# Folding two weight matrices with split fp32r matmuls instead of fp32 ones, beside a routing chain, in a fused attention and mixture-of-experts kernel

## The chip, the cores and the metric

The kernel runs on one NeuronCore of a Trainium2 chip. The metric is the device time of one execution in microseconds, as the median of several runs. The engines are called PE (TensorE, the matrix engine; PEld is its weight load), ACT (ScalarE), DVE (VectorE), POOL (GpSimd) and SP (SyncE, which here only issues DMAs).

## What is computed

Three layers in a row, all float32:

```
S = 768, B = 4, H = 8, D = 48            # linear attention with decay
for t in range(S):
    y[t]  = r[t] @ (state + (u*k[t]) outer v[t])
    state = w * state + k[t] outer v[t]
x = y as [3072, 384]                     # tokens by features
skip   = x @ w_skip <= 0                 # such tokens pass unchanged
e      = argmax(x @ w_gate)              # one of 8 experts
x     += softmax(x @ w_gate)[e] * (relu(x @ w1[e]) @ w2[e])
out    = (((x @ wm1) * (x @ wm2)) @ w3) @ w_out     # w3 1024x1024, w_out 1024x384
```

The kernel never multiplies a token by w3: it first computes the product w3 @ w_out ("the fold"), 1024x384, and multiplies by that.

## The kernel before

The program has three stages on the time axis: attention (0 to about 121 us), routing (about 122 to 155 us: which token goes to which slot of which expert), experts (to about 291 us), and the gated layers (to the end). All five instruction queues run through them without a barrier between the first three.

**The fold** (class `Fold`, lines 40 to 102) is spread over the end of attention, the routing, and the seams of the experts, to give PE work while it would wait for others. It goes by chunks of 128 rows of w3, i = 0 to 7. For each: `load` (SP, line 59) brings the chunk into one of three buffers `w3_in`; `turn` (PE, line 69) transposes it in eight pieces into two PSUM banks; `turned` (ACT, line 77) copies these to `w3T` as float32 in two halves of 512 columns; `product` (PE, line 84) multiplies the eight pieces of `w3T` by the eight row blocks of w_out (`wo`) and sums in one bank, 128x384; it can be called by quarters of two pieces; `taken` (ACT, line 99) copies the result to `wf`. `product` uses plain fp32 matmuls, which the trace shows as two records each, so 16 for a product. Chunk 0 is turned and multiplied in attention, chunks 1 to 4 and half of 5 in the routing, the rest later.

**The rest of the kernel** uses "split" operands where it multiplies: ACT writes the fp32r rounding of a value (`hi`), DVE subtracts it from the value and writes the remainder (`lo`), and PE does three fp32r matmuls, hi by hi, hi by lo, lo by hi. So do the experts (line 1277 first layer, line 1293 second layer, the latter with 128x128 stationary and 384 moving columns) and the gated layers (lines 1523 and 1538).

**The order of work around the change** is written out by hand, one queue per engine:

- SP: behind attention's last stores of x it waits for the last logits (`s_lg`, line 286), loads chunk 3, stores the last part of x (line 288), loads chunk 4 (line 800), waits for the summed logits, loads expert 0's w1 (line 802), chunks 5 and 6, expert 0's w2, and then, after the gates have been transposed, stores the list of gates and loads chunk 7.
- PE in attention (lines 430 to 437): turns chunk 0 and 1 and multiplies product 0 between attention's last steps. In routing (lines 829 to 863): turn 2, product 1 quarters 0 to 2, the counts (lines 833 to 840, they wait for a scan on DVE, line 919), product 1 quarter 3, turn 3, the transposes of the gates, product 2, turn 4, product 3 quarters 0 to 2, the list of tokens (lines 850 to 856, it waits for DVE's one-hot tensors `oh_lo`, line 949, and ACT's `vals`, line 876), product 3 quarter 3, turn 5, product 4 in two parts around turn 6, turn 7, half of product 5. Then expert 0's transposes, which wait for the gathered tokens (line 1258), the other half of product 5 (line 1306), and expert 0's hidden layer.
- DVE in routing (lines 908 to 963): one chain of small operations, each of which waits for the one before, from the logits to `slot_token` (line 954), from which POOL gathers the tokens (line 824); then the low parts of expert 0's w1 (line 957).
- POOL in routing: one comparison, two memsets, and then it waits for `slot_token`.
- ACT in routing (lines 866 to 884): the exponential of the logits, and `turned` and `taken` in turn with the gates' copy, `vals` and the high parts of expert 0's w1 (line 879).

Of the kernel before, what the change touches and what calls it, by code (L numbers as in the profile page):

```python
# [12 lines left out]
P = 128  # L13
# [20 lines left out]
LINE = 1024  # L34
# [5 lines left out]
class Fold:  # L40
# [3 lines left out]


    def __init__(self, nc, sb, sem, ident, s_ident, w3, w_out):
# [4 lines left out]
        self.w3T = [sb(f"w3T{i}", [P, self.KF, P]) for i in range(3)]  # L51
# [4 lines left out]
        self.s_T, self.s_Tout = sem("fold_T"), sem("fold_Tout")  # L56
# [11 lines left out]

    def turn(self, pe, i, banks):

        wait(pe, self.s_w3[i % 3], 16 * (i // 3 + 1))
        wait(pe, self.s_Tout, 2 * i)
        for g in range(self.KF):
            m = pe.transpose(banks[g // 4][:, (g % 4) * P:(g % 4 + 1) * P], self.w3_in[i % 3][:, g * P:(g + 1) * P], self.ident[:, :])
        m.then_inc(self.s_T, 1)

    def turned(self, act, i, banks):

        wait(act, self.s_T, i + 1)
        wait(act, self.s_W, i - 2)  # L80
        for h in range(2):
            act.activation(flat(self.w3T[i % 3][:, 4 * h:4 * h + 4, :]), banks[h][:, :], ACT.Copy).then_inc(self.s_Tout, 1)

    def product(self, pe, i, bank, quarters=(0, 1, 2, 3)):

        if 0 in quarters:
            wait(pe, self.s_Tout, 2 * i + 2)
            wait(pe, self.s_Wout, i - 1)
        n = self.KF // 4
        for q in quarters:  # L90
            for g in range(q * n, (q + 1) * n):
                if i == 0 and g % (self.KF // 2) == 0:
                    pe.wait_ge(self.s_wo[g // (self.KF // 2)], 16)
                m = pe.matmul(bank[:, 0:self.DM], self.w3T[i % 3][:, g, :], self.wo[:, g, :],  # L94
                              start=(g == 0), stop=(g == self.KF - 1), skip_group_check=True)
# [19 lines left out]
def attention(nc, env, sem, r, k, v, w, u, xbuf):  # L115
# [16 lines left out]
    with ExitStack() as ctx:  # L132
# [120 lines left out]
        def _(sp):  # L253
# [32 lines left out]
            sp.wait_ge(s_lg, 1)  # L286
            fold.load(sp, [3])
# [156 lines left out]
        def _(act):  # L444
# [83 lines left out]
        def _(dve):  # L528
# [83 lines left out]
            schedule(dve, ((masks, 0), (states, -1), (bonuses, 1), (rT_out, 1), (x_out, -1), (k_decay, 2)), 2, 1, extra)  # L612
            dve.wait_ge(s_lg, 1)
# [114 lines left out]
def routing(nc, env, NT, E, NSL, CAP, ROOM, xbuf):  # L728
# [8 lines left out]
    with ExitStack() as ctx:  # L737
# [20 lines left out]
        pos = sb("pos", [P, E, NT])  # L758
        over = sb("over", [P, E, NT])
# [39 lines left out]
        def _(sp):  # L799
            fold.load(sp, [4])  # L800
# [12 lines left out]
        def _(pool):  # L813
# [16 lines left out]
        def _(pe):  # L830
# [18 lines left out]
            fold.product(pe, 3, p_W[1], (0, 1, 2))  # L849
# [7 lines left out]
            fold.product(pe, 3, p_W[1], (3,))  # L857
# [29 lines left out]
        def _(dve):  # L887
# [63 lines left out]

            dve.wait_ge(s_list, 1)
# [785 lines left out]
```

## Time and profile before

| | |
|---|---|
| median of 3 runs | 608.86 us (608.21 to 608.92) |
| the profiled execution | 608.56 us, its span 606.8 us |
| mean granted clock of PE | 0.996 |
| PE busy | 589.0 us, 97% of the span |
| DVE, ACT, POOL busy | 295.1, 226.7, 156.3 us |
| the chain that ended last | 92% on PE, 3% on DVE, 1% on DMA |
| moved by DMA | 67.80 MB, 112 GB/s on average |

The span is the time from the first to the last instruction of one execution; the time of the execution has some 1.8 us more around it. Times of rows are microseconds from the start of the span, unless marked ns. "Busy" is the time in which an engine had at least one instruction under way; matmuls overlap in the pipeline, so the busy time of one matmul (0.34 us for 384 columns) is longer than the step from one to the next (0.174 us). In the chain of work, each piece lasts until the next piece of the chain begins, so there these steps can be read.

### The profile page before, as it was taken

Reading aid. Unit: us, or ns where it says so; the run is one execution under the profiler, and the core shown is the slowest. Engines: PE = TensorE matmul, PEld = TensorE weight load, DVE = VectorE, ACT = ScalarE, POOL = GpSimd, SP = SyncE. Lnnn points to the kernel's source line nnn. Section 1 sums busy time; section 2 is a strip of 40 time slices with the busy share of each in tenths; the row PEclk is TensorE's granted clock in tenths of the full one; section 3 lists DMA queues with packets and bytes.
Section 4 is the critical chain, followed back from the end, with each engine's and each line's share of the span. In section 5 each row is a group of like instructions: output and inputs, shape, how many; then the busy total and the mean of one; then the engine's idle time right before and its main releaser. Section 6 shows DMA issues by size and latency. Waiting matters only on the chain.

```text
span 606.8 us, 17257 instructions
## 1 busy us (share of the span) xinstructions
PE 589.0 (97%) x7295; PEld 526.0 (87%) x7295; DVE 295.1 (49%) x474; ACT 226.7 (37%) x410; POOL 156.3 (26%) x179
## 2 busy tenths in 40 slices
PE   6699999999999999999999999999999999999997
PEld 6689999766999999999688888888888888888886
DVE  5478889283677777784124233322413323332212
ACT  3156666445655555653143122222213222222212
POOL 7568788214154444441150000000000000000000
PEclk9899999999999999999999999999999999999999
DMA  7779998686467776650350021004004001001001
GB/s 132 133 140 183 184 186 188 226 278 240 175 255 277 279 271 250 204 187 20 100 79 1 1 74 31 0 9 97 0 1 104 1 0 53 1 0 51 2 1 52
DMA packets 133218, 67.80 MB, mean 112 GB/s; under 512 B 111228, under 2 KB 127232, under 8 KB 133176
## 3 DMA queue, kind: packets, MB, share of 16 engines
q1 hardware_dynamic: 105320, 57.91, 33.3%
q10 hardware_dynamic: 25552, 4.72, 4.2%
q0 software_dynamic: 2304, 4.59, 2.2%
q8 instruction: 28, 0.46, 0.3%
q14 instruction: 14, 0.11, 0.1%
HBM read 55.92 MB, written 12.20 MB: 112 GB/s over the span
## 4 chain that ended last, share of the span: by engine, by line
PE 92%; DVE 3%; issue 2%; DMA 1%; ACT 0%; DVEq 0%; POOL 0%; SPq 0%; POOLq 0%
PE gl_pab L1523 33%; PE p_pair L1293 11%; PE ex_ph L1277 11%; PE gl_po L1538 8%; PE p_pair L1538 8%; PE p_pair L94 5%; PE p_K L293 2%; PE p_Y L359 2%; PE p_pair L406 2%; PE p_Y L380 2%; PE p_Y L338 2%; PE p_R L293 2%; PE p_pair L374 2%; DVE k_dec L600 1%; DMA w_in<-xbuf 1%
## 5 line engine op out<-in xcount | busy, mean ns | idle before, releaser
L1612 DVE TENSOR_TENSOR gl_g_sb<-gl_a_sb,gl_pab 128x512 f32<-128x512 f32 x48 | 33.0, 688 | 173.9 <-ACT gl_a_sb L1574 173.9
L1523 PE MATMUL gl_pab<-gl_xT_hi,wm_lo 128*128 128x512 f32 x288 | 113.0, 393 | 0.0
L1523 PE MATMUL gl_pab<-gl_xT_lo,wm_hi 128*128 128x512 f32 x288 | 112.9, 392 | 0.0
L1523 PE MATMUL gl_pab<-gl_xT_hi,wm_hi 128*128 128x512 f32 x288 | 112.2, 390 | 0.0
L1574 ACT ACTIVATE gl_a_sb<-gl_pab 128x512 f32<-128x512 f32 x48 | 28.7, 597 | 186.1 <-PE gl_pab L1523 186.1
L1523 PEld LDWEIGHTS gl_pab<-gl_xT_hi,wm_lo 128*128 128x128 f32 x288 | 54.0, 188 | 11.4
L1523 PEld LDWEIGHTS gl_pab<-gl_xT_hi,wm_hi 128*128 128x128 f32 x288 | 54.1, 188 | 10.5 <-DVE gl_xT_lo L1619 0.3
L1523 PEld LDWEIGHTS gl_pab<-gl_xT_lo,wm_hi 128*128 128x128 f32 x288 | 54.0, 188 | 10.4
L1277 PE MATMUL ex_ph<-ex_xT_hi,ew_w_hi 128*128 128x224 f32 x192 | 52.9, 276 | 0.0
L1277 PE MATMUL ex_ph<-ex_xT_hi,ew_w_lo 128*128 128x224 f32 x192 | 52.7, 275 | 0.0
L1277 PE MATMUL ex_ph<-ex_xT_lo,ew_w_hi 128*128 128x224 f32 x192 | 52.7, 274 | 0.0
L1614 DVE TENSOR_TENSOR gl_g_lo<-gl_g_sb,gl_g_hi 128x512 fp32r<-128x512 f32 x48 | 33.2, 692 | 33.5 <-ACT gl_g_hi L1577 33.5
L1577 ACT ACTIVATE gl_g_hi<-gl_g_sb 128x512 fp32r<-128x512 f32 x48 | 30.3, 632 | 36.2 <-DVE gl_g_sb L1612 36.2
L1293 PE MATMUL p_pair<-ew_w_hi,ex_h_hi 128*96 128x384 f32 (+1 forms) x128 | 43.5, 340 | 0.0
L1293 PE MATMUL p_pair<-ew_w_hi,ex_h_lo 128*96 128x384 f32 (+1 forms) x128 | 43.1, 336 | 0.0
L1293 PE MATMUL p_pair<-ew_w_lo,ex_h_hi 128*96 128x384 f32 (+1 forms) x128 | 43.0, 336 | 0.0
L1043 POOL DMA_INDIRECT ew_x_in<-xbuf,slot_token x16 | 22.4, 1403 | 71.0 <-DVE ex_x_new L1404 49.9
L94 PE MATMUL p_pair<-wo,w3T 128*128 128x384 f32 x112 | 38.8, 490 | 0.5 <-PEq L1701 0.4
L1277 PEld LDWEIGHTS ex_ph<-ex_xT_hi,ew_w_hi 128*128 128x128 f32 x192 | 36.9, 192 | 0.2
L1277 PEld LDWEIGHTS ex_ph<-ex_xT_lo,ew_w_hi 128*128 128x128 f32 x192 | 36.9, 192 | 0.1
L1277 PEld LDWEIGHTS ex_ph<-ex_xT_hi,ew_w_lo 128*128 128x128 f32 x192 | 36.9, 192 | 0.0
L1339 ACT ACTIVATE ew_w_hi<-ew_w_in 128x768 fp32r<-128x768 f32 x32 | 26.9, 840 | 18.2 <-PE p_pair L1293 18.2
(200 smaller groups left out, 1226.5 us busy)
## 6 DMA issues: line engine op xcount, KB each, us to landing
w_in<-in_moe_w SPq DMA_DIRECT2D x8, 1536.0 KB, 7.6
ew_w_in<-in_moe_w SPq DMA_DIRECT2D x8, 1536.0 KB, 6.6
w_in<-in_moe_w SPq DMA_DIRECT2D x14, 512.0 KB, 7.3
k_in<-in_k SPq DMA_DIRECT2D x48, 96.0 KB
v_in<-in_v ACTq DMA_DIRECT2D x48, 96.0 KB
r_in<-in_r SPq DMA_DIRECT2D x48, 96.0 KB
out<-gl_o_sb SPq DMA_DIRECT2D x12, 384.0 KB, 2.7
w_in<-xbuf SPq DMA_DIRECT2D x60, 64.0 KB, 2.4
```

The source lines that it names most:

```text
L94: m = pe.matmul(bank[:, 0:self.DM], self.w3T[i % 3][:, g, :], self.wo[:, g, :], start=(g == 0), stop=(g == self.KF - 1), skip_group_check= ...
L293: return pe.transpose(out, x, ident[rows, rows])
L1043: pool.indirect_dma_start(self.x_in[slot][0:tokens.shape[0], i, :], None, xbuf[:, :], bass.IndirectOffsetOnAxis(ap=tokens, axis=0), bounds ...
L1277: m = pe.matmul(p_h[g][:, f % 2, 0:width(t)], a[:, k, cols], b[:, k, 0:width(t)], start=(k == 0 and n == 0), stop=(k == KD - 1 and n == 2))
L1293: m = pe.matmul(p_y[i][0:n_tok, 0:DM], a[:, f, cols], b[:, f, :], start=(f == 0 and n == 0), stop=(f == KF - 1 and n == 2))
L1339: act.activation(flat(w2_hi[:, 2 * g:2 * g + 2, :]), flat(w2_in[:, 2 * g:2 * g + 2, :]), ACT.Copy).then_inc(s_w2hi, 1)
L1523: m = pe.matmul(p_ab[f % 2][w][:, :], a[:, w * KD + k, cols], b[t.slot][:, k, :], start=(k == 0 and n == 0), stop=(k == KD - 1 and n == 2))
L1538: m = pe.matmul(p_o[i][:, 0:DM], a[f % 2][:, cols], b[:, f, :], start=(f == 0 and n == 0), stop=(f == KF - 1 and n == 2))
L1574: act.activation(a_sb[f % 2][:, :], p_ab[f % 2][0][:, :], ACT.Copy).then_inc(s_a, 1)
L1577: act.activation(g_hi[f % 2][:, :], g_sb[f % 2][:, :], ACT.Copy).then_inc(s_ghi, 1)
L1612: dve.tensor_tensor(g_sb[f % 2][:, :], a_sb[f % 2][:, :], p_ab[f % 2][1][:, :], ALU.mult).then_inc(s_g, 1)
L1614: dve.tensor_tensor(g_lo[f % 2][:, :], g_sb[f % 2][:, :], g_hi[f % 2][:, :], ALU.subtract).then_inc(s_glo, 1)
```

## The change

Products 1 to 5 use split operands. Products 0, 6 and 7 stay fp32.

- ACT splits w_out: `wo_hi` in four parts of 768 columns, three behind attention's last y_out, the fourth behind `turned(1)`. DVE writes `wo_lo` in four parts behind its last work of attention.
- `turned(i)` for i = 1 to 5 writes the fp32r rounding `hi` instead of the float32 value. The remainder `lo`, in two halves of 512 columns: for chunks 1, 4 and 5 by DVE from PSUM (`rest_dve`). For chunks 2 and 3 ACT copies the float32 value out too (two more copies of 512 columns), and POOL subtracts from SBUF (`rest_pool`), for chunk 3 only after `s_slot`, which DVE gives when `oh_hi` is done.
- DVE does chunk 1's remainder before the last logits, chunk 4's between the one-hot tensors and the wait for the list, chunk 5's in the middle of the low parts of w1.
- `product` does 24 fp32r matmuls for 1 to 5 and waits for the halves of `lo` and the parts of `wo_lo` it uses. Product 3 is done as a whole before the list of tokens.
- SP loads chunks 3 and 4 as soon as their buffers are free and stores the last part of x when it has been kept, both ahead of the last logits.
- The new tiles lie over memory that is free at their time: `wo_hi`, `wo_lo` where expert 0's w2_hi, w2_lo come later (so ACT waits for product 5 before it writes w2_hi), `hi[1]`, `lo` at the top of SBUF. `pos` and `over` share memory with `key` and `dif`.

The diff, cut to its core:

```diff
+    RAW = {0: 0, 2: 1, 3: 0, 6: 0, 7: 1}
+    BY_POOL = (2, 3)
+    BY_DVE = (1, 4, 5)
...
+    def out_hi(self, act, q):
+        rows = slice(2 * q, 2 * q + 2)
+        act.wait_ge(self.s_wo[q // 2], 16)
+        act.activation(flat(self.wo_hi[:, rows, :]), flat(self.wo[:, rows, :]), ACT.Copy).then_inc(self.s_wohi, 1)
+
+    def out_lo(self, dve, q):
+        rows = slice(2 * q, 2 * q + 2)
+        dve.wait_ge(self.s_wohi, q + 1)
+        dve.tensor_tensor(flat(self.wo_lo[:, rows, :]), flat(self.wo[:, rows, :]), flat(self.wo_hi[:, rows, :]), ALU.subtract).then_inc(self.s_wolo, 1)
...
     def turn(self, pe, i, banks):
         wait(pe, self.s_Tout, 2 * i)
+        if i in (4, 5):
+            wait(pe, self.s_raw, 2 * (i - 3))
+        if i in (2, 6, 7):
+            wait(pe, self.s_dlo, {2: 2, 6: 4, 7: 6}[i])
...
     def turned(self, act, i, banks):
         wait(act, self.s_T, i + 1)
-        wait(act, self.s_W, i - 2)
+        if i in (0, 6, 7):
+            wait(act, self.s_plo, {0: 0, 6: 4, 7: 2}[i])
+            for h in range(2):
+                act.activation(self.half(self.w3T[self.RAW[i]], h), banks[h][:, :], ACT.Copy).then_inc(self.s_Tout, 1)
+            return
+        wait(act, self.s_W, i - 1 if i > 2 else 0)
         for h in range(2):
-            act.activation(flat(self.w3T[i % 3][:, 4 * h:4 * h + 4, :]), banks[h][:, :], ACT.Copy).then_inc(self.s_Tout, 1)
+            act.activation(self.half(self.hi[i % 2], h), banks[h][:, :], ACT.Copy).then_inc(self.s_Tout, 1)
+        if i in self.BY_POOL:
+            for h in range(2):
+                act.activation(self.half(self.w3T[self.RAW[i]], h), banks[h][:, :], ACT.Copy).then_inc(self.s_raw, 1)
+
+    def rest_dve(self, dve, i, banks):
+        for h in range(2):
+            dve.wait_ge(self.s_Tout, 2 * i + h + 1)
+            dve.tensor_tensor(self.half(self.lo[i % 2], h), banks[h][:, :], self.half(self.hi[i % 2], h), ALU.subtract).then_inc(self.s_dlo, 1)
+
+    def rest_pool(self, pool, i):
+        for h in range(2):
+            pool.wait_ge(self.s_raw, 2 * (i - 2) + h + 1)
+            pool.tensor_tensor(self.half(self.lo[i % 2], h), self.half(self.w3T[self.RAW[i]], h), self.half(self.hi[i % 2], h), ALU.subtract).then_inc(self.s_plo, 1)
...
     def product(self, pe, i, bank, quarters=(0, 1, 2, 3)):
...
+                if i in self.BY_POOL:
+                    wait(pe, self.s_plo, 2 * (i - 2) + h + 1)
+                if i in self.BY_DVE:
+                    wait(pe, self.s_dlo, 2 * self.BY_DVE.index(i) + h + 1)
...
+                for n3, (a, b) in enumerate(((hi, self.wo_hi), (hi, self.wo_lo), (lo, self.wo_hi))):
+                    m = pe.matmul(bank[:, 0:self.DM], a[:, g, :], b[:, g, :],
+                                  start=(g == 0 and n3 == 0), stop=(g == self.KF - 1 and n3 == 2), skip_group_check=True)
...
-            sp.wait_ge(s_lg, 1)
-            fold.load(sp, [3])
+            fold.load(sp, [3, 4])
+            wait(sp, s_kept, BASE + NT)
             store_x(sp, env, xbuf, 1, 2, NCH - 2)
...
+                if f is y_out and at(c, j, NT):
+                    for q in range(3):
+                        fold.out_hi(act, q)
                 if f is y_out and at(c, j, NT + 2):
                     fold.turned(act, 1, [p_R[:, i, :] for i in range(2)])
+                    fold.out_hi(act, 3)
...
+            for q in range(3):
+                fold.out_lo(dve, q)
+            fold.rest_dve(dve, 1, [p_R[:, i, :] for i in range(2)])
+            fold.out_lo(dve, 3)
             dve.wait_ge(s_lg, 1)
...
-            fold.load(sp, [4])
             sp.wait_ge(env["s_logits"], 1)
...
+            fold.rest_pool(pool, 2)
+            pool.wait_ge(s_slot, 1)
+            fold.rest_pool(pool, 3)
             pool.wait_ge(s_clear, 4)
...
-            fold.product(pe, 3, p_W[1], (0, 1, 2))
+            fold.product(pe, 3, p_W[1])
             pe.wait_ge(s_near, 1)
...
-            fold.product(pe, 3, p_W[1], (3,))
...
+            fold.rest_dve(dve, 4, p_T[0])
             dve.wait_ge(s_list, 1)
...
-            ex.first_w1_lo(dve)
+            ex.first_w1_lo(dve, (0, 1))
+            fold.rest_dve(dve, 5, p_T[1])
+            ex.first_w1_lo(dve, (2, 3))
...
             def w2_part(t, g):
+                if g == 0 and is_first(t):
+                    act.wait_ge(fold.s_W, 6)
```

## Rows read from the trace of the kernel before

**Rows 1.** The page, part 1: busy us, share of the span, instructions of each engine.
```profile
PE 589.0 (97%) x7295; PEld 526.0 (87%) x7295; DVE 295.1 (49%) x474; ACT 226.7 (37%) x410; POOL 156.3 (26%) x179
```

**Rows 2.** Table by stretches: from:to, us; busy us per engine; clock, DMA share, GB/s.
```profile
156.00:290.00 134.00, 134.00 (x994) 131.50 (x994) 96.70 (x127) 73.44 (x112) 55.81 (x39) 1.00 0.57 205
290.00:304.00 14.00, 13.47 (x52) 8.42 (x51) 2.21 (x4) 2.71 (x6) 1.08 (x2) 1.00 0.44 107
```

**Rows 3.** The chain of work, in order: start us, us until the next, what.
```profile
122.71 3.87 PE p_pair L94 x12
...
129.73 5.16 PE p_pair L94 x16
134.89 0.87 PE ro_pT L74 x8
...
139.64 0.86 PE ro_p_list L854 x24
140.50 1.36 PE p_pair L94 x4
...
155.43 8.03 PE ex_ph L1277 x72
```

**Rows 4.** The chain of work, first half of expert 2's second layer.
```profile
197.44 4.21 PE p_pair L1293 x24
```

**Rows 5.** Timeline of DVE: start us, us, what [idle before, and what ended it].
```profile
125.57 0.56 DVE L919 TENSOR_TENSOR_SCAN ro_earlier<-tb_mine,tb_restart 128x192 bf16<-128x192 bf16 x1 [0.15 <-DVE tb_mine L895]
...
128.18 0.17 DVE L931 TENSOR_TENSOR_SCAN ro_ends<-tb_one,ro_n_blocks 128x8 f32<-128x8 f32 x1
...
132.56 1.16 DVE L795 TENSOR_TENSOR ro_vals<-ro_oh_hi,tb_first 128x960 bf16<-128x960 bf16 x1
...
134.06 3.43 DVE L949 TENSOR_TENSOR ro_oh_lo<-tb_col,ro_lo 128x1536 bf16<-128x1536 bf16 x2
```

**Rows 6.** Timeline of ACT, 117 to 139 us.
```profile
117.31 0.49 ACT L501 ACTIVATE xT<-p_K 128x384 f32<-128x384 f32 x1 [2.48 <-PE p_K L293]
...
124.37 1.07 ACT L82 ACTIVATE w3T<-ro_pT 128x512 f32<-128x512 f32 x2
...
138.22 3.04 ACT L1035 ACTIVATE ew_w_hi<-w_in 128x768 fp32r<-128x768 f32 x4 [1.33 <-DMA w_in<-in_moe_w]
```

**Rows 7.** Timeline of DVE before the logits, and at expert 0's w1.
```profile
122.02 0.57 DVE L615 TENSOR_TENSOR lg<-lg_parts 128x216 f32<-128x216 f32 x1 [7.92 <-ACT lg_parts L508]
...
141.12 3.57 DVE L1038 TENSOR_TENSOR ew_w_lo<-w_in,ew_w_hi 128x768 fp32r<-128x768 f32 x4
```

**Rows 8.** Timeline of SP's DMA issues: start us, us, what.
```profile
122.01 0.33 SPq L62 DMA_DIRECT2D w_in<-in_moe_w  x1
...
126.36 2.24 SPq L1026 DMA_DIRECT2D w_in<-in_moe_w  x1
```

**Rows 9.** DVE and POOL: two lines (ns min/median/max), then both timelines.
```profile
L1499 POOL TENSOR_TENSOR gl_wf_lo<-wf,gl_wf_hi x8: 1007/1016/1501, 303.8 to 311.2; 128x384 fp32r<-128x384 f32 x8
...
L600 DVE TENSOR_TENSOR k_dec<-k_in,k_pow x24: 548/629/1232, 8.7 to 104.3; 128x384 f32<-128x384 f32 x24
...
100.13 0.55 DVE L584 TENSOR_TENSOR x_nat<-p_R,v_bonus 128x384 f32<-128x384 f32 x1
100.59 1.23 DVE L600 TENSOR_TENSOR k_dec<-k_in,k_pow 128x384 f32<-128x384 f32 x1
104.33 0.96 DVE L600 TENSOR_TENSOR k_dec<-k_in,k_pow 128x384 f32<-128x384 f32 x1
309.64 0.69 DVE L1614 TENSOR_TENSOR gl_g_lo<-gl_g_sb,gl_g_hi 128x512 fp32r<-128x512 f32 x1 [0.70 <-ACT gl_g_hi L1577]
...
99.80 0.82 POOL L662 TENSOR_TENSOR state<-state_sum,w_sq 128x384 f32<-128x384 f32 x1
100.59 0.82 POOL L669 TENSOR_TENSOR v_bonus<-v_in,bonus 128x384 f32<-128x384 f32 x1
104.06 1.93 POOL L669 TENSOR_TENSOR v_bonus<-v_in,bonus 128x384 f32<-128x384 f32 x2
```

More of the change, by code:

```diff
@@ L40, with __init__ @@
 class Fold:
-    def __init__(self, nc, sb, sem, ident, s_ident, w3, w_out):
+    RAW = {0: 0, 2: 1, 3: 0, 6: 0, 7: 1}
+    BY_POOL = (2, 3)
+    BY_DVE = (1, 4, 5)
+    def __init__(self, nc, sb, sem, at, top, ident, s_ident, w3, w_out):
         FM, DM = w_out.shape
@@ L50, in __init__ @@
         self.w3_in = [sb(f"w3_in{i}", [P, FM]) for i in range(2)]
-        self.w3T = [sb(f"w3T{i}", [P, self.KF, P]) for i in range(3)]
+        self.w3T = [sb(f"w3T{i}", [P, self.KF, P]) for i in range(2)]
+        shape = [P, self.KF, P]
+        self.hi = [sb("w3T_hi0", shape, F32R), at("w3T_hi1", shape, F32R, top - 3 * 4 * FM)]
+        self.lo = [at(f"w3T_lo{i}", shape, F32R, top - (2 - i) * 4 * FM) for i in range(2)]
         self.wo = sb("wo", [P, self.KF, DM])
@@ L90, in product @@
         for q in quarters:
+            h = q // 2
+            if q % 2 == 0:
+                wait(pe, self.s_Tout, 2 * i + h + 1)
+                if i in self.BY_POOL:
+                    wait(pe, self.s_plo, 2 * (i - 2) + h + 1)
+                if i in self.BY_DVE:
+                    wait(pe, self.s_dlo, 2 * self.BY_DVE.index(i) + h + 1)
+            if i == 1:
+                pe.wait_ge(self.s_wolo, q + 1)
             for g in range(q * n, (q + 1) * n):
@@ L757, in routing @@
         earlier = sb("earlier", [P, E * NT], BF16)
-        pos = sb("pos", [P, E, NT])
-        over = sb("over", [P, E, NT])
+        pos, over = key, dif
         is_over = sb("is_over", [P, E, NO])
@@ L1061, in first_w1_hi, with first_w1_lo @@
             self.split_w1_hi(act, g)
-    def first_w1_lo(self, dve):
-        for g in range(self.NG):
+    def first_w1_lo(self, dve, parts):
+        for g in parts:
             dve.wait_ge(self.s_w1hi, g + 1)
@@ L1674, in program, with at @@
         s_iota = sem("s_iota")
+        def at(n, s, d, offset):
+            return nc.alloc_sbuf_tensor_at(n, s, d, offset=offset)
         ident = sb("ident", [P, P])
@@ L1681, in program @@
             "w_gate": moe_w_gate, "w_skip": moe_w_skip, "wm": (moe2_w1, moe2_w2),
-            "fold": Fold(nc, sb, sem, ident, s_iota, moe2_w3, moe2_w_out),
+            "fold": Fold(nc, sb, sem, at, nc.sbuf_usable_end // LINE * LINE, ident, s_iota, moe2_w3, moe2_w_out),
             "s_wmlo": sem("s_wmlo"), "lg": sb("lg", [P, E + 1, N // P]), "seq": S,
@@ L1696, in program @@
         env["p_pair"] = c.enter_context(nc.psum_tensor("p_pair", [P, 2, 512], F32))
+        behind = nc.sbuf_base + 5 * 4 * KD * FM
+        env["fold"].wo_hi, env["fold"].wo_lo = (at(n, [P, FM // P, DM], F32R, behind + i * 4 * DM * FM // P) for i, n in enumerate(("wo_hi", "wo_lo")))
         with ExitStack() as ce:
```

16 lines of the change are left out of this document (11 added, 5 removed).

## Prediction, made before the changed kernel was run

> **What bounds the kernel now.** I read the page's busy shares first: TensorE (PE) is busy for 97% of the span and the others for half or less [rows 1]. A mean hides stages, so the table by stretches comes next: through the experts PE is busy in every microsecond, and its clock is granted in full [rows 2]. The chain of work that ended last says the same for the place that is edited: from 122.71 to 155.43 us it runs along PE alone, product by product, with no wait in it (the pieces left out are the counts, transposes and products of the same kinds) [rows 3]. So a microsecond of PE work taken out of this stretch is worth a microsecond at the end, as long as nothing else becomes late; the experts behind it follow each other without a gap, and the scatter and reload behind them hang on their end. The question is therefore twofold: how much PE work goes, and which of the new operations on ScalarE (ACT), VectorE (DVE) and GpSimd (POOL) comes too late.
>
> **What a product costs, before and after.** A product of the fold is 8 fp32 matmuls, which the trace shows as 16 records; the chain gives 5.16 us for such a product, 0.32 us a record [rows 3]. The new form is 24 fp32r matmuls with a 128x128 stationary and 384 moving columns. The experts' second layer runs exactly this, high by high, high by low, low by high, and the chain gives 4.21 us for 24 of them, 0.174 us each [rows 4]. So each of products 1 to 5 gets shorter by 0.97 us: 4.85 us in all. Products 0, 6 and 7 stay as they are.
>
> **Before the counts most of product 1's gain is lost.** Three quarters of product 1 take 3.87 us and end at 126.58; then come the counts [rows 3]. As 18 fp32r matmuls they take 3.13 us and end at 125.84. But the counts also wait for DVE's scan, which ends at 126.13 [rows 5]; the trace has the weight load of the counts released by DVE. Counts start about 126.3 instead of 126.59: 0.3 us won, 0.4 us lost to a new wait. The last quarter gives 0.3 us more, so product 2 starts at about 129.15 instead of 129.73 and product 2 (4.2 instead of 5.16 us) and the transposes of chunk 4 (0.87 us [rows 3]) end at 134.2 instead of 135.76: 1.56 us ahead.
>
> **Parts that I cost at nothing, with their cover.**
> - The three early high copies of w_out (ACT, 768 columns): four of this size take 3.04 us, so 2.3 us for three [rows 6]. ACT has 2.48 us of idle time just there [rows 6]. The cover is tight; without it two copies for x slip by a few tenths. The fourth (0.8 us) lies behind turned(1), which ends about 119.4 (turn 1 ends at 118.3, and a pair of copies takes 1.07 us), over 2 us ahead of the last logits.
> - The four low parts and the two halves of chunk 1's remainder on DVE: 4 x 0.87 + 2 x 0.6 us = 4.7 us [rows 7], the subtraction of 512 columns taken from g_lo, 0.69 us with its overlap [rows 9]. They start behind the high copies, about 115.6, and end about 121.3, inside an idle stretch of DVE of 7.92 us that ends at 122.02 [rows 7]. Cover left: 0.7 us. If it went, the logits and the whole routing chain would go with it.
> - The second pair of copies in turned(2) and turned(3): ACT runs such a pair in 1.07 us [rows 6]. Behind it wait taken(1) and the copy of the gates, about 0.6 us later than before; SP's store of the gate list follows, and DVE needs the gates only behind expert 0's second layer, over 30 us on.
> - SP: the loads of chunks 3 and 4 go from 122.01 and behind the stores to about 116 and 118.3, when turns 0 and 1 have freed their buffers, the last stores of x, which stood behind the load at 122.01, to about 119, and the first w1 load, queued behind them all, from 126.36 to about 122.6 [rows 8]. ACT now idles 1.33 us for that load [rows 6]; it will find it there. Nothing is moved later on this queue but the load of chunk 6, by PE's own time of turning chunk 3, which is earlier.
> - Chunk 4's remainder on DVE (two times 0.6 us) stands behind the one-hot work and before the wait for the list; the list takes 0.86 us of PE, so slot_token may come 0.4 us later than it could. The gather behind it on POOL has room: expert 0's transposes come 12 us behind the list, behind PE's own half of product 5, and the chain has no wait for the gathers there [rows 3]. If they came too late, the delay would go into the end one for one. Chunk 5's remainder sits among the w1 splits, each needed only after 150 us.
> - The wait for product 5 ahead of the w2 split: taken(5) on the same queue waits for that already. The moved tiles cost no instruction.
>
> **POOL and DVE.** This is the term that decides. POOL gets two subtractions of 512 columns for chunk 2 and two for chunk 3. The same operation on 384 columns takes 1.016 us and steps at 0.98 [rows 9]; in proportion 512 take 1.3 us. All operands lie in SBUF, and the trace shows what that does to DVE: its product k_dec, with two SBUF inputs, takes 0.55 us alone, but 1.23 us when a POOL product of 0.82 us starts with it [rows 9]. It stands still for the whole POOL operation (0.68 of 0.82 us; the rest is its start-up). A DVE operation that reads PSUM, x_nat at 100.13, keeps its 0.55 us beside a POOL product [rows 9]. The other way round POOL waits: its subtraction takes 1.501 us at most, and the long one is the one in which DVE's g_lo ran, itself at 0.69 us [rows 9]. And at 104.33 a k_dec got in between two POOL products instead of behind both [rows 9]. So the one that starts first holds, the other stands still, and they take turns. The Trainium skill, SBUF — State Buffer, section "Who interferes with whom", has the same: a DVE instruction with two SBUF inputs and a GpSimd instruction that reads SBUF exclude each other for a whole instruction. By that rule alone I would not know the turns; these come from 104.33.
>
> First place: chunk 2's remainder runs on POOL from 126.1 (its raw copy lands at about 125.95) to 128.7, ahead of product 2 at 129.15. DVE's short scan at 128.18 has two SBUF inputs [rows 5] and waits for the end of it, 0.5 us, and with it the chain up to oh_hi: s_slot, given just ahead of slot_values at 132.56 [rows 5], comes at 132.9 instead of 132.4.
>
> Second place: chunk 3's remainder starts at s_slot, beside slot_values (1.16 us) and the two one-hot operations (3.43 us) [rows 5], which all read SBUF twice. If DVE gets in first: slot_values to 134.1, POOL's first half to 135.4, one-hot to 137.1, second half to 138.4, one-hot to 140.0. Product 3 (PE is ready at 134.2) then starts at 135.5, stops at its middle until 138.4 and ends at 140.5. If POOL gets in first: first half to 134.3, slot_values to 135.4, second half to 136.7, one-hots to 140.0; product 3 runs 134.3 to 136.4 and 136.7 to 138.8, and PE waits for the one-hots until 140.0. Either way the matmuls of the list start at L = 140.0 to 140.5 instead of 138.4, which the shorter products alone would give.
>
> **The sum.** Before, the list starts at 139.64 and the last quarter of product 3 (1.36 us) stands behind it [rows 3]; after, it stands ahead. Products 4 and 5 give 1.95 us. Gain = (139.64 - L) + 1.36 + 1.95 = 142.95 - L. With L = 140.25 it is 2.7 us. The profiled execution took 608.56 us (span 606.8), 0.3 us under the median of the three runs, 608.86. 608.56 - 2.7 = 605.9; halfway towards the median, I say 606.0.
>
> The unseen prices: DVE work in bf16 with broadcast inputs beside POOL. Bounds from the rows: nothing (like DVE operations that read PSUM) and standing still for all of POOL's time (k_dec). I take the second, the nearest in kind. No gain can come of it.
>
> **Rivals.**
> 1. The two engines hardly disturb each other here. For it: the one-hots read broadcast bf16, a few bytes only. Against: v_bonus also reads a broadcast input, on POOL, and still stopped k_dec. Then L = 138.4 and the gain is 4.5 us: 604.0.
> 2. POOL doesn't get its turn until DVE is through, because DVE's operations follow each other closely (as at 309.64, where DVE slipped in between two of POOL). One-hots end at 138.0, POOL's halves at 139.2 and 140.5, L = 143.3 with product 3 started at 139.2 (two halves of 2.08 us): 608.9, no change. Against it: 104.33, where POOL's and DVE's waiting instructions alternate.
> 3. Slower: the same place with a dearer POOL operation. If each half costs what the slowest row allows (1.501 us for 384 columns, 2.0 us for 512), chunk 2's remainder ends at 130.1 and holds DVE's scan until then, s_slot comes at 134.3, and starved as in 2 the second half ends at 143.4 and L is 145.6: 611.2. It decides from the point where L passes 142.95 (loss at all) or 144.2 (over 0.2%).
> 4. The change doesn't do what it says: 24 fp32r matmuls in the place of 16 fp32 records give nothing, for instance from switching between both kinds around each transpose. Then only the new waits are left: 609 to 610. Against it: the experts' 24 [rows 4], between whose halves fp32 transposes stand as well.
>
> **How the numbers follow.** Forecast 0.54; rival 1, or a part of it, 0.22; rival 2 0.09; rival 3 0.05; rival 4 0.03; something outside these (a load of SP, a DMA that is late) 0.07, of which I give two thirds to no change or slower. A measurement of this kernel can tell about 0.2%, 1.2 us, from no change. Faster by more than that (under 607.6): the forecast, rival 1 and a part of the rest, 0.80. Same: 0.12. Slower: 0.08. The range of 8 in 10 runs from rival 1 with a little to spare, 603.8, to a forecast with half of its gain lost once more, 608.0; rivals 2 to 4 stay outside.
>
> **What would show it.** Right: products 1 to 5 at 4.2 us each and the first expert's hidden layer at about 152.7 instead of 155.43; PE idle just ahead of the counts; one or two one-hot operations, or slot_values, at about 3 us instead of 1.76 (or 1.16) beside POOL's subtractions; PE waiting for POOL's remainder in product 3 or for the one-hots before the list. Wrong: one-hots of 1.76 us with POOL at 1.3 us beside them (rival 1), POOL's subtractions of 3 us and more (rivals 2 and 3), products of 5 us (rival 4), or a logits chain that ends after 122.6 because the cover on DVE or ACT was too thin, which would take its delay from the gain one for one. A granted clock under 1.00 behind the new gaps would also prove it wrong; the stretch from 290 us, in which PE idles 0.5 us in all, has the full clock [rows 2].

## The result, and the profile after

The changed kernel takes 605.47 us (median of 5 runs, 604.85 to 606.1), the kernel before 608.86 us (5 runs on the same chip, 608.21 to 609.06): a ratio of 0.9941, with a 95% interval of 0.9925 to 0.9957. It is faster, by 3.4 us; I had said 606.0. The same kernel run again (e10 below, on the chip of e9 and e11) took 605.13 us (6 runs), a ratio of 0.9942 [0.9926, 0.9958]. The profiled execution of the changed kernel took 604.85 us, with a span of 603.1 us, against 608.56 and 606.8 before.

The page's part 1 answers to [rows 1]:

```profile
PE 584.7 (97%) x7335; PEld 531.8 (88%) x7335; DVE 303.8 (50%) x484; ACT 231.6 (38%) x418; POOL 162.7 (27%) x183
```

The table by stretches answers to [rows 2] (from:to, us; busy us per engine; clock, DMA share, GB/s):

```profile
122.00:130.00 8.00, 7.58 (x52) 6.94 (x51) 6.76 (x20) 4.31 (x10) 4.28 (x7) 1.00 1.02 346
130.00:140.00 10.00, 9.15 (x69) 8.59 (x68) 9.65 (x11) 7.15 (x12) 3.45 (x2) 1.00 0.95 363
140.00:150.00 10.00, 10.00 (x80) 9.91 (x77) 6.78 (x14) 3.79 (x8) 5.35 (x5) 1.00 0.18 52
156.00:286.00 130.00, 130.00 (x960) 127.53 (x959) 94.84 (x125) 71.50 (x109) 55.77 (x39) 1.00 0.58 207
```

PE has 4.3 us less to do, the other three engines 5 to 9 us more. PE is no longer busy in every microsecond: it idles 0.42 us from 122 to 130 and 0.85 us from 130 to 140. Those are the two new waits that show as idle time; two short ones hide in PE's steps and are told below. The clock stays at 1.00 behind them, and from 156 us on PE is busy throughout, as before.

The chain of waits of this profile goes back only to about 296 us, so the edited stretch is read from PE's timeline (start us, us, what [idle before, and what ended it]; of each product the first matmul stands). It answers to [rows 3]:

```profile
121.33 1.09 PE L97 MATMUL ro_pT<-ident,w_in 128*128 128x128 f32 x8
122.18 0.42 PE L154 MATMUL p_pair<-wo_hi,w3T_hi 128*128 128x384 f32 x1
...
125.97 0.26 PE L904 MATMUL ro_p_count<-tb_mine,tb_before 128*128 128x192 bf16 x1 [0.41 <-DVEq L988]
...
128.81 0.42 PE L154 MATMUL p_pair<-wo_hi,w3T_hi 128*128 128x384 f32 x1
...
133.08 1.03 PE L97 MATMUL ro_pT<-ident,w_in 128*128 128x128 f32 x8
134.01 0.41 PE L154 MATMUL p_pair<-wo_hi,w3T_hi 128*128 128x384 f32 x1
...
138.35 0.61 PE L923 MATMUL ro_p_list<-ro_vals,ro_oh_lo 128*128 128x80 bf16 x12
139.81 0.60 PE L923 MATMUL ro_p_list<-ro_vals,ro_oh_lo 128*128 128x80 bf16 x12 [0.85 <-DVE ro_oh_lo L1017]
140.24 1.06 PE L97 MATMUL ro_pT<-ident,w_in 128*128 128x128 f32 x8
...
152.00 0.28 PE L1348 MATMUL ex_ph<-ex_xT_lo,ew_w_hi 128*128 128x224 f32 x1
```

L97 lines are the transposes (turns 2, 4 and 5), L154 the split products, L904 the counts, L923 the list. Product 2 takes from 128.81 to 133.08, 4.27 us instead of 5.17 us. Product 3 starts 0.93 us behind turn 4, in e1 below, where nothing on POOL has to be waited for, 0.79 us: it waits 0.14 us for POOL's first half, which ends at 133.87. At its middle, where POOL's second half has just ended (136.04), it loses another 0.09 us that e1 doesn't lose: the record at 136.18 is followed at 136.44, its neighbours after 0.174 us.

**Where the 3.7 us of span went.** Whole executions differ ahead of this stretch, so I cut each trace into parts, by starts that every trace has: turn 2 (121.33 above), the second record of the first expert's hidden layer (152.00), the last `ex_x_new`, the first gated matmul, the end. All starts here and below are those of the timelines; the chain's are up to 0.2 us later at some places.

| part, us | before | after | difference |
|---|---|---|---|
| start to turn 2 | 121.62 | 121.33 | -0.29 |
| turn 2 to hidden layer (**the stretch**) | 33.75 | 30.67 | **-3.08** |
| hidden layer to last `ex_x_new` | 135.52 | 135.50 | -0.02 |
| to the first gated matmul (reload of x) | 12.26 | 11.92 | -0.34 |
| to the end | 303.65 | 303.68 | +0.03 |

The part ahead of turn 2 varied from 120.07 to 123.72 us between the profiles of this study, and from 120.99 to 123.72 among kernels that are alike up to there; the difference of two profiles says nothing about it. The stretch is a sharp instrument: 30.67 in after and 30.69 when it was run again. The reload part has two levels: 11.92 to 12.03 us in eight of the profiles, 12.22 to 12.26 in five, which are before and the four kernels below in which POOL doesn't do chunk 3 (e1, e3, e4, e9), but not e7, in which it doesn't either. It is 0.3 us, and whether the change has a part in it was not settled.

### The profile page after: what moved, and what is told of

The parts are those of the page before. It is cut to its first block, busy times and chain, and to the rows that moved or that the text cites. A ratio compares the mean times of both kernels' runs of the same rounds, so it can differ in the third digit from the quotient of the medians.

```text
span 603.1 us, 17367 instructions
## 1 busy us (share of the span) xinstructions
PE 584.7 (97%) x7335; PEld 531.8 (88%) x7335; DVE 303.8 (50%) x484; ACT 231.6 (38%) x418; POOL 162.7 (27%) x183
## 4 chain that ended last, share of the span: by engine, by line
PE 50%; DVE 0%; ACT 0%; issue 0%
PE gl_pab L1596 33%; PE gl_po L1611 8%; PE p_pair L1611 8%; PE p_pair L149 0%; PE gl_pab L1585 0%; DVE gl_g_lo L1687 0%; DVE gl_g_sb L1685 0%; ACT gl_g_hi L1650 0%; ACT gl_a_sb L1647 0%; DVE gl_o_sb L1709 0%
## 5 line engine op out<-in xcount | busy, mean ns | idle before, releaser
L1611 PE MATMUL gl_po<-gl_wf_hi,gl_g_hi 128*128 128x384 f32 x96 | 32.7, 341 | 0.7 <-DVE gl_g_lo L1687 0.7
```

The source lines that it names most:

```text
L1611: m = pe.matmul(p_o[i][:, 0:DM], a[f % 2][:, cols], b[:, f, :], start=(f == 0 and n == 0), stop=(f == KF - 1 and n == 2))
```

## The two places where DVE meets POOL

DVE and POOL in after, second place (it answers to [rows 5]):

```profile
131.29 1.16 DVE L963 TENSOR_TENSOR ro_oh_hi<-tb_col,ro_hi 128x960 bf16<-128x960 bf16 x1
132.60 2.29 DVE L862 TENSOR_TENSOR ro_vals<-ro_oh_hi,tb_first 128x960 bf16<-128x960 bf16 x1
134.81 1.27 DVE L1013 TENSOR_SCALAR ro_lo_i<-ro_dest_i 128x24 int32<-128x24 int32 x1
...
136.32 3.43 DVE L1017 TENSOR_TENSOR ro_oh_lo<-tb_col,ro_lo 128x1536 bf16<-128x1536 bf16 x2
...
132.59 3.45 POOL L128 TENSOR_TENSOR w3T_lo<-w3T,w3T_hi 128x512 fp32r<-128x512 f32 x2 [4.34 <-DVEq L1011]
```

POOL's first half begins 0.01 us ahead of slot_values (L862), and slot_values takes 2.29 instead of 1.16 us: it stood still. POOL's second half took 2.22 us where an undisturbed one takes 1.28, so it stood still while slot_values really ran, and then held the small `ro_lo_i`: 1.27 us for 24 integers. The one-hots (L1017) begin only behind both and are not disturbed. They end at 139.75, and PE's second half of the list waits for that.

At the first place POOL's remainder of chunk 2 ran beside the small operations of the routing:

```profile
125.72 2.52 POOL L128 TENSOR_TENSOR w3T_lo<-w3T,w3T_hi 128x512 fp32r<-128x512 f32 x2 [1.58 <-ACT w3T L116]
...
126.66 0.38 DVE L992 TENSOR_SCALAR ro_g_r<-ro_g_r 128x24 f32<-128x24 f32 x1
...
128.21 0.17 DVE L999 TENSOR_TENSOR_SCAN ro_ends<-tb_one,ro_n_blocks 128x8 f32<-128x8 f32 x1
```

One half is 1.26 us; the second ended at 128.24, and the scan at 128.21 kept its 0.17 us. Only the operation at 126.66 was held: it takes 0.38 instead of 0.18 us and ends just behind POOL's first half (126.98). A further 0.11 us is lost between `ro_is_over` (127.52) and the operation after it (127.92): 0.40 us from start to start, 0.29 in before and in e7, in which POOL does nothing there. What takes it was not settled.

## Experiments

All are the changed kernel with one edit, but for e7, which is before with one edit. "Stretch" is the time from turn 2 to the hidden layer, 33.75 us before and 30.67 us after.

**e1, chunk 3's remainder is gone.** POOL's two subtractions are left out, with PE's waits for them (not shown), and product 3 reads an old `lo`.

```diff
-            pool.wait_ge(s_slot, 1)
-            fold.rest_pool(pool, 3)
```

> The changed kernel without GpSimd's two subtractions for chunk 3 (product 3 multiplies a stale remainder, so chunk 3's part of the fold is only rounded; the number of matmuls is the same). My theory: GpSimd's two operations make VectorE stand still for 1.1 us each, once in slot_values (2.29 us) and once in the tiny lo_i (1.27 us). Without them these take 1.16 and 0.17 us, the one-hots end at 137.5 instead of 139.75, PE goes from product 3 into the list without its wait of 0.85 us, and the time is 0.8 us below the changed kernel's (605.5 to 604.7). Rival: GpSimd is not the cause (bf16 or broadcast inputs, or the chain before it): slot_values and lo_i stay long and the time stays at 605.5.

603.83 us (4 runs), ratio 0.9924 [0.9906, 0.9942]; stretch 29.43 us, 1.24 less than after. DVE, then PE:

```profile
133.13 1.16 DVE L862 TENSOR_TENSOR ro_vals<-ro_oh_hi,tb_first 128x960 bf16<-128x960 bf16 x1
134.21 0.17 DVE L1011 TENSOR_SCALAR ro_lo_i<-ro_dest_i 128x24 int32<-128x24 int32 x1
...
134.62 3.43 DVE L1015 TENSOR_TENSOR ro_oh_lo<-tb_col,ro_lo 128x1536 bf16<-128x1536 bf16 x2
...
133.62 1.03 PE L97 MATMUL ro_pT<-ident,w_in 128*128 128x128 f32 x8
134.41 0.42 PE L154 MATMUL p_pair<-wo_hi,w3T_hi 128*128 128x384 f32 x1
...
138.66 1.03 PE L921 MATMUL ro_p_list<-ro_vals,ro_oh_lo 128*128 128x80 bf16 x24
```

Both stretched operations are back at 1.16 and 0.17 us, with nothing else changed on DVE: it is POOL's work beside them that held them, and the two stops cost 1.13 and 1.10 us. The list runs as one piece of 24. Of the 1.24 us, 1.02 are the list (0.87 instead of 1.89 us to turn 5); the rest is product 3, which no longer waits for POOL's first half (0.14 us) and no longer stops at its middle for the second (0.09 us). I had expected 0.8 us, the wait at the list alone. The time of the whole, 603.83 us, is near the 604.0 that rival 1 of the prediction gave to a DVE that nothing holds.

**e2, POOL starts only behind the one-hots.** This makes rival 2 of the prediction on purpose.

```diff
-            pool.wait_ge(s_slot, 1)
+            pool.wait_ge(s_token, 3)
             fold.rest_pool(pool, 3)
```

> GpSimd begins chunk 3's subtractions only when VectorE has finished the one-hots (the wait for slot is a wait for the last token). This forces the case of my second rival. My theory: VectorE is undisturbed (slot_values 1.16, lo_i 0.17, one-hots end at 137.5), GpSimd's halves take 1.26 us each and end at 138.8 and 140.0, product 3 waits on PE for 4.7 us and runs 138.8 to 143.0, the list ends at 143.9 instead of 140.4, and the time is 3.4 us above the changed kernel's: 608.9, equal to the kernel before. Rival: the start of product 3 is not bound by the remainder alone, and the delay shows only in part: 1 us or less.

611.77 us (4 runs), ratio 1.0056 [1.0038, 1.0075]; stretch 36.48 us. The rival had been priced at 608.9. PE's timeline:

```profile
139.06 0.66 PE L154 MATMUL p_pair<-wo_hi,w3T_hi 128*128 128x384 f32 x1 [4.90 <-POOL w3T_lo L128]
...
140.16 0.53 PE L154 MATMUL p_pair<-wo_hi,w3T_hi 128*128 128x384 f32 x1
140.48 0.53 PE L154 MATMUL p_pair<-wo_lo,w3T_hi 128*128 128x384 f32 x1
...
145.25 1.03 PE L923 MATMUL ro_p_list<-ro_vals,ro_oh_lo 128*128 128x80 bf16 x24
```

The table by stretches of the same kernel:

```profile
130.00:140.00 10.00, 5.10 (x30) 4.86 (x30) 8.38 (x13) 6.68 (x12) 2.35 (x2) 0.82 0.95 353
140.00:150.00 10.00, 10.00 (x76) 9.81 (x74) 3.50 (x7) 1.58 (x3) 2.09 (x3) 0.84 0.04 8
```

Product 3 starts at 139.06, where the rival had it (139.2), but it takes 6.19 us instead of 4.34. Behind 4.90 us of idle PE the granted clock is 0.82 and 0.84 in the two stretches, and the matmuls from 139.52 to 143.04 follow each other every 0.32 us, which is 384 columns at the lower of the two levels, 1.2 GHz; in after, and in e2 itself behind 143.33, the step is 0.174. Against after, counted from turn 2: 4.97 us of later start, 1.85 us of slower product, and 1.02 us off for the list, which has nothing to wait for now: 5.80 us, measured 5.81.

**e11, the same with a busy PE.** Forty transposes of the identity stand in the gap, to take the clock out of e2 and keep the wait.

```diff
             fold.turn(pe, 4, p_T[0])
+            pe.wait_ge(fold.s_raw, 4)
+            keep_warm(pe, fold.ident, p_T[1][0], 40)
             fold.product(pe, 3, p_W[1])
```

> The run with GpSimd's late start, and 40 transposes of the identity on PE in the place where it stood waiting for GpSimd (4.9 us); nothing else. In the run without them product 3 took 6.2 us instead of 4.3, at a granted clock of 0.82 to 0.84 of full speed in the two stretches of 10 us from there. My theory: the clock fell because PE did nothing; with the transposes product 3 takes 4.2 to 4.3 us at full clock and the time falls by 1.9 us, from 611.8 to 609.9. Rival: product 3 was slow because its operands or VectorE's and GpSimd's work beside it slowed it, and it stays at 6 us.

609.49 us (10 runs), ratio 1.0008 [0.9996, 1.002]; stretch 34.57 us, 1.91 less than e2. PE's timeline:

```profile
134.46 4.53 PE L31 MATMUL ro_pT<-ident 128*128 128x128 f32 x40
...
139.53 0.41 PE L154 MATMUL p_pair<-wo_hi,w3T_hi 128*128 128x384 f32 x1 [0.54 <-POOL w3T_lo L128]
...
143.78 1.03 PE L925 MATMUL ro_p_list<-ro_vals,ro_oh_lo 128*128 128x80 bf16 x24
```

The table by stretches of the same kernel:

```profile
130.00:140.00 10.00, 9.46 (x73) 9.21 (x72) 8.80 (x14) 7.16 (x12) 1.90 (x2) 1.00 0.98 372
140.00:150.00 10.00, 10.00 (x84) 9.81 (x83) 4.97 (x8) 2.67 (x5) 3.74 (x4) 1.00 0.11 32
```

The clock is 1.00 throughout and product 3 takes 4.25 us again, with the same operations on DVE and POOL beside it; e11's own rival, that these slow product 3, is out. So rival 2's price had two parts, the wait, about what I had worked out, and 1.9 us of clock, which I had left out.

**e3, DVE does chunk 3's remainder.** It reads PSUM, as for the other chunks, right behind `s_slot`; POOL and the two extra copies of ACT are not needed for it. The waits of the later turns are fitted to that (not shown).

```diff
-    BY_POOL = (2, 3)
-    BY_DVE = (1, 4, 5)
+    BY_POOL = (2,)
+    BY_DVE = (1, 3, 4, 5)
...
             dve.sem_inc(s_slot, 1)
+            fold.rest_dve(dve, 3, p_T[1])
```

> Chunk 3's remainder by VectorE from PSUM, right behind the slot semaphore; GpSimd has only chunk 2, and ScalarE's second pair of copies for chunk 3 is gone. My theory: VectorE pays 1.25 us for its own two subtractions in the place of 2.2 us of standing still; product 3's first half is ready at about 133.3, the one-hots end at 138.7, PE waits 0.0 to 0.3 us in the list instead of 0.85, and the time is 0.5 to 0.8 us below the changed kernel's. Rival: the work on VectorE costs the chain as much as GpSimd's did: no difference.

604.6 us (4 runs), ratio 0.9935 [0.9914, 0.9956]; stretch 29.61 us, 1.06 less than after. DVE's timeline:

```profile
133.10 1.29 DVE L122 TENSOR_TENSOR w3T_lo<-ro_pT,w3T_hi 128x512 fp32r<-128x512 f32 x2
134.31 1.15 DVE L862 TENSOR_TENSOR ro_vals<-ro_oh_hi,tb_first 128x960 bf16<-128x960 bf16 x1
...
135.79 3.43 DVE L1016 TENSOR_TENSOR ro_oh_lo<-tb_col,ro_lo 128x1536 bf16<-128x1536 bf16 x2
```

Doing the work costs DVE 1.21 us; leaving it to POOL cost it 2.2 us of standing still. The engine that is to be relieved does better by doing the work itself. The stretch gains 1.06 us where 0.5 to 0.8 was expected: the list costs 1.07 us instead of 1.89, and product 3 no longer waits for POOL. POOL's whole instruction is lost to DVE, and POOL needs 1.26 us for a half that DVE does in 0.6.

**e4, product 3 stays fp32.** No remainder is needed for it.

```diff
-    BY_POOL = (2, 3)
+    BY_POOL = (2,)
...
-                if i in (0, 6, 7):
+                if i in (0, 3, 6, 7):
                     m = pe.matmul(
```

> Product 3 stays fp32 with its plain copy, products 1, 2, 4, 5 are split; GpSimd has only chunk 2. My theory: product 3 takes 5.16 us again (1.0 us more on PE), but the one-hots end at 137.5, so the wait of 0.85 us at the list is gone: the time is within 0.3 us of the changed kernel's, which says that splitting product 3 brings next to nothing in this order. Rival: the wait at the list has another cause and stays: 1.0 us slower.

605.07 us (5 runs), ratio 0.9947 [0.9929, 0.9965]; stretch 30.39 us, 0.28 less than after. Product 3 takes 5.17 us (134.75 to 139.92), and the list behind it waits for nothing. So in the changed kernel the split of product 3 wins nothing; with its remainder on POOL it costs 0.28 us more than it saves. The time of the runs can't tell these two kernels apart, the stretch can.

**e5 and e6, the transposes of the next chunk fill the gaps.** e5 puts turn 5 between product 3 and the list. e6 also puts turn 3 ahead of the counts.

```diff
             fold.product(pe, 3, p_W[1])
+            fold.turn(pe, 5, p_T[1])
             pe.wait_ge(s_near, 1)
...
             m.then_inc(s_list, 1)
-            fold.turn(pe, 5, p_T[1])
```

> One step on PE moved: the transposes of chunk 5 go ahead of the list of tokens instead of behind it. Their operands have been there for long. My theory: the wait of 0.85 us at the list's second half is filled by the 0.87 us of transposes, the list still ends at about 140.4, and product 4 starts there instead of at 141.06: 0.8 us below the changed kernel's. Rival: the list ends later by the same 0.87 us and so do slot_token and the gathers, and the gain is lost: no difference.

604.97 us (6 runs), ratio 0.9942 [0.9925, 0.9958]; stretch 30.08 us, 0.59 less than after. From the list's start at 139.96 to product 4 at 141.24 it takes 1.28 us instead of 0.87. The expectation of 0.8 us left out that the next step has a wait of its own: product 4 needs chunk 4's remainder, which DVE begins only behind the one-hots:

```profile
139.96 1.20 PE L924 MATMUL ro_p_list<-ro_vals,ro_oh_lo 128*128 128x80 bf16 x24
...
140.41 1.28 DVE L122 TENSOR_TENSOR w3T_lo<-ro_pT,w3T_hi 128x512 fp32r<-128x512 f32 x2
```

The list is busy for 1.20 us (1.03 where it waits for nothing, as in e1), so some 0.2 of the 0.41 us are its own wait for the one-hots, and the rest lies between it and product 4. The trace doesn't name the releaser of the second part.

> As the run before, and the transposes of chunk 3 go ahead of the counts. They fill the 0.41 us that PE waits for VectorE's scan; the counts then start 0.45 us later than in the changed kernel, about 126.4, and end at 127.1, before VectorE asks for them at 127.5. My theory: 0.4 us more, so 1.2 us below the changed kernel's, about 604.3. Rival: VectorE's chain is late by what the counts are late (0.45 us), the one-hots with it, and the list gives the 0.4 us back: no better than the run before.

605.05 us (6 runs), ratio 0.9938 [0.9919, 0.9956]; stretch 30.05 us, no better than e5, where I had expected 0.4 us more. The wait ahead of the counts is gone, and comes back one step on, in the timelines of PE and POOL:

```profile
136.37 0.41 PE L154 MATMUL p_pair<-wo_hi,w3T_hi 128*128 128x384 f32 x1 [0.47 <-POOL w3T_lo L128]
...
134.96 3.44 POOL L128 TENSOR_TENSOR w3T_lo<-w3T,w3T_hi 128x512 fp32r<-128x512 f32 x2 [4.34 <-DVEq L1011]
```

The counts come 0.3 us later with turn 3 ahead of them, but that doesn't delay DVE's chain. (The rival in the expectation, which forecast this time, said that it would.) POOL starts chunk 3's remainder 11.24 us behind turn 2, in after 11.26. PE is at product 3 earlier, and POOL's first half comes when it came before, so product 3 starts 12.65 us behind turn 2, in after 12.68. In after it already started straight behind that half. Time saved on PE is kept only when what PE waits for next comes earlier too.

**e9, the three together.** The edit of e3, and both moved transposes of e6.

> Chunk 3's remainder on VectorE (as in the run that did this alone), the transposes of chunk 3 ahead of the counts and those of chunk 5 ahead of the list. From PE's transposes of chunk 2 to expert 0's hidden layer the changed kernel takes 30.67 us, the run with VectorE alone 29.61. My theory: the first move fills the 0.41 us before the counts, and this time it is kept, since product 3's remainder no longer starts so late that product 3 waits for it; the second fills the 0.2 us that the list still takes too long. 29.0 us for the stretch and 1.6 us below the changed kernel's time, about 603.9. Rival: the moves give what they gave with GpSimd, nothing beyond one of them, and the stretch stays at 29.6.

603.93 us (6 runs), ratio 0.9917 [0.9902, 0.9933]; stretch 29.04 us, 1.63 less than after, with the expectation at 29.0. PE and DVE:

```profile
126.60 1.04 PE L97 MATMUL ro_pT<-ident,w_in 128*128 128x128 f32 x8
127.47 0.25 PE L903 MATMUL ro_p_count<-tb_mine,tb_before 128*128 128x192 bf16 x1
...
138.87 1.03 PE L97 MATMUL ro_pT<-ident,w_in 128*128 128x128 f32 x8
139.74 1.02 PE L922 MATMUL ro_p_list<-ro_vals,ro_oh_lo 128*128 128x80 bf16 x24
...
133.79 1.29 DVE L122 TENSOR_TENSOR w3T_lo<-ro_pT,w3T_hi 128x512 fp32r<-128x512 f32 x2
...
136.48 3.43 DVE L1016 TENSOR_TENSOR ro_oh_lo<-tb_col,ro_lo 128x1536 bf16<-128x1536 bf16 x2
```

No line of PE in the stretch shows a wait; two short ones hide in its steps, 0.15 us ahead of product 3 and 0.05 us ahead of product 4. With DVE's first half done 0.69 us behind its start at 133.79, product 3 starts 12.09 us behind turn 2 instead of 12.68, so the first move is kept here. The one-hots end at 139.91, the list's first half covers the rest. Measured together with before and the changed kernel (0.9942), this is the fastest that computes the whole: 4.9 us under before, 1.2 under the changed kernel. The intervals of the two ratios overlap; the stretch says 1.63 us.

**e7 and e8, the loads.** e7 is before with the new order of SP alone, e8 is after with the old order of SP.

```diff
-            sp.wait_ge(s_lg, 1)
-            fold.load(sp, [3])
+            fold.load(sp, [3, 4])
+            wait(sp, s_kept, BASE + NT)
             store_x(sp, env, xbuf, 1, 2, NCH - 2)
...
-            fold.load(sp, [4])
             sp.wait_ge(env["s_logits"], 1)
```

> The kernel before with only SP's new order: chunks 3 and 4 load as soon as their buffers are free, x is stored when kept. My theory: PE waited for no load there, so the time is the kernel before's within 0.3 us, though w1 lands earlier and ScalarE's wait of 1.33 us for it goes. Rival: the loads were part of the gain (0.5 us or more faster).

608.12 us (10 runs), ratio 0.9998 [0.9986, 1.0009]; stretch 33.75 us, the same as before's to the hundredth. The early loads alone do nothing.

> The changed kernel with SP's old order of loads and stores. My theory: turn 3 asks for chunk 3 at 127.8, 0.7 us earlier than before, and turn 4 for chunk 4 at 133.1; both landed earlier than that in the kernel before. w1 lands at about 138, ScalarE's high parts of w1 end at 141.3 instead of 138.2, and turned(5) stands behind them; product 4's start does not depend on it, turn 6 waits for turned(5) at most a few tenths. Time within 0.4 us of the changed kernel's. Rival: the split products need the early loads, and it is 1 us or more slower.

605.3 us (8 runs), ratio 0.9949 [0.9936, 0.9963]; stretch 30.67 us, the same as after's. But here I had taken the loads to be in time, and they are not (PE's timeline):

```profile
132.54 1.09 PE L97 MATMUL ro_pT<-ident,w_in 128*128 128x128 f32 x8 [0.56 <-DMA w_in<-in_moe_w]
...
138.54 0.60 PE L924 MATMUL ro_p_list<-ro_vals,ro_oh_lo 128*128 128x80 bf16 x12 [0.25 <-DVE ro_oh_lo L1018]
```

Turn 4 waits 0.56 us for chunk 4, and the list's wait shrinks from 0.85 to 0.25 us: PE arrives later at a place where it would have waited anyway. The early loads are worth nothing in the changed kernel only because the one-hots are the later of the two. In e9 that wait is gone and turn 4 starts 11.15 us behind turn 2, while chunk 4 let it start only 12.47 us behind in e8. By my estimate from these two the early loads are worth up to 1.3 us there; that kernel with the old order was not run.

**e10** is the changed kernel once more, on the chip of e9 and e11.

> The changed kernel once more, as it is, on the same chip as the combined one, to compare the two directly. The ratio to the kernel before is again 0.994 to 0.995; its stretch from chunk 2's transposes to expert 0 takes 30.7 us, whatever the stage ahead of it takes (which moved by over 1 us from run to run).

605.13 us (6 runs); stretch 30.69 us.

## Why the prediction was right, point by point

The result, 605.47 us, lies 0.5 us from the forecast, on the side of more gain. By its steps, with the numbers of after moved by 0.29 us so that turn 2 falls together with before's:

- **What bounds the kernel**: right. In e1, e3, e5 and e9 what was taken from PE's path or its waits came out as a shorter stretch, and the experts behind it kept 135.5 us in all.
- **The price of a product**: 4.2 us forecast; 4.27 (product 2), 4.34 (product 3, with 0.09 us lost at its middle), 4.25 in e11. The products' own step is the 0.174 us of [rows 4]. What is over is at the start: the first record of each product is followed after 0.26 us instead of 0.174. That is so behind fp32 transposes, but also behind the bf16 counts (126.65, 126.91) and behind the wait inside product 3 (136.18, 136.44), so it is not the switch from transposes alone; its cause stays open. From turn 5 to the hidden layer, products 4 and 5 gave 13.67 - 11.76 = 1.91 us; forecast 1.95. The prediction took 0.97 us a product where its own rows, 5.16 - 4.21, give 0.95. Rival 4 is excluded: e4, with product 3 back in fp32, takes 5.17 us for it, e1 with the split one 4.25.
- **The counts**: 126.3 forecast, 126.26 measured, with PE's wait of 0.41 us for DVE's scan (forecast 0.4). Product 2 at 129.10 (129.15), product 3 at 134.30, where PE was forecast to be ready at 134.2 and POOL's first half done at 134.3: it did wait for POOL, by the 0.14 us above. The hidden layer's second record at 152.29 (152.7).
- **The covers**: all held. ACT wrote the three high copies in 2.31 us (forecast 2.3) and was at its next copy in time; DVE's low parts and chunk 1's remainder ended at 120.85 us, and 0.88 us of idle time were left before the logits (forecast 0.7); the w1 load was there when ACT came to it, so the 1.33 us of [rows 6] are gone. ACT and DVE:

```profile
114.63 2.31 ACT L81 ACTIVATE wo_hi<-wo 128x768 fp32r<-128x768 f32 x3
117.03 0.49 ACT L561 ACTIVATE xT<-p_K 128x384 f32<-128x384 f32 x1
...
135.13 3.05 ACT L1106 ACTIVATE ew_w_hi<-w_in 128x768 fp32r<-128x768 f32 x4
...
119.89 0.96 DVE L86 TENSOR_TENSOR wo_lo<-wo,wo_hi 128x768 fp32r<-128x768 f32 x1
121.73 0.56 DVE L683 TENSOR_TENSOR lg<-lg_parts 128x216 f32<-128x216 f32 x1 [0.88 <-ACT lg_parts L568]
```

- **POOL's price**: 1.3 us a half forecast by proportion from 384 to 512 columns, 1.26 to 1.28 measured. With that, rival 3 (2.0 us a half) had no ground.
- **The lock**: the likeliest case happened, in its form "POOL gets in first". Moved to before's time: POOL's first half ends at 134.2 (forecast 134.3), slot_values at 135.2 (135.4), POOL's second half at 136.3 (136.7), the one-hots at 140.04 (140.0). The unseen price of bf16 work beside POOL was taken from k_dec [rows 9], and it held: DVE stands still for the whole operation. That POOL's second half met the tiny `ro_lo_i` and not the first one-hots, as forecast, changes nothing in the sum: the one-hots begin behind it either way. e1 shows the cause, and rival 1 is out. The rule cited in the prediction (the Trainium skill, SBUF — State Buffer, "Who interferes with whom") agrees with slot_values at 2.29 us; the same section also names copies, casts and `tensor_scalar` as able to take the shared ports where their operands meet its conditions, and `ro_lo_i` at 1.27 us agrees with that.
- **Right in size by luck**: the first place. I let the scan wait 0.5 us for POOL. It came 0.3 us late for other reasons, just as POOL's second half was ending (128.21 and 128.24), and did not wait. What was slowed was the `tensor_scalar` at 126.66, by 0.2 us, and the step behind `ro_is_over`, by 0.1 us. ACT's part of the values, which starts when `oh_hi` is done, came 11.21 us behind turn 2 instead of 10.89: 0.3 us for all of it, where 0.5 was forecast, by another mechanism.
- **Mis-sized: the list.** I put all 0.86 us of the list behind the end of the one-hots. But the list is two halves, each behind its own half of the one-hots: the first ran at 138.35, straight behind product 3, and only the second (0.43 us) stood behind the wait. That is 0.43 us. The forecast L was the middle of 140.0 and 140.5, and the second half began at 140.1, 0.15 us early; the chain's times, which I subtracted from, are 0.16 us later than the timeline's starts at this place, which takes it back; products 4 and 5 gave 0.04 less. 2.70 + 0.43 + 0.15 - 0.16 - 0.04 = 3.08, the measured gain of the stretch.
- **Rival 2** was given 608.9 and, made on purpose, took 611.77. The failed term is the length of product 3 behind the gap: I used 4.2 us, it is 6.19. I had named a clock under 1.00 behind the new gaps as a thing that would prove me wrong; gaps of 0.41 and 0.85 us left it at 1.00, one of 4.90 did not. A rival with a long idle PE in it must be priced at the lower clock.
- **The loads** cost nothing, as forecast (e7), and bring nothing in the changed kernel (e8); e8 shows that the second is the luck of two waits in a row and not slack in the loads.

Of the 3.4 us of the medians, 3.1 are thus explained by the stretch. The remaining 0.3 us lie within what the part ahead of turn 2 and the reload vary by.

## What to carry to other kernels

Before work is given to POOL to relieve DVE, add up what each POOL instruction will hold up on DVE: here 1.21 us of work were spared and 2.2 us of standing still were paid, and DVE doing it itself from PSUM (e3) gave 1.06 us back. A wait that a later wait covers hides the worth of everything ahead of it (e6, e8), so remove the last one first and then measure the rest again. Where runs vary by more than the change, compare a stretch that starts and ends at records which every kernel has.

## What the runs showed of the hardware that I had not expected

- A `tensor_scalar` of 24 integers per partition, with a single input, stands still beside a POOL subtraction like one with two inputs: 1.27 us in after, 0.17 in e1, e3 and e9. Here the smallest operation paid as much as the large one before it (1.10 and 1.13 us).
- After 4.90 us without a matmul, PE's granted clock was 0.82 and 0.84 in the two stretches of 10 us around the restart, and product 3 took 1.85 us longer. Forty fp32 transposes in the gap kept the clock at 1.00 (e11) and took all of that back.
- With the lock, DVE and POOL alternated, instruction by instruction: in the same 3.5 us DVE waited twice for POOL and POOL once for DVE.
